# Asking for a slot's first weights four tiles sooner, and making a table's first loads depend on the expert

## The reference

```python
x = filter(x)                                  # (14336, 192)
for layer in (0, 1):
    e = argmax(x @ w_gate[layer])              # one of 8 experts per token
    h = relu(x @ w1[layer][e])                 # 192 -> 1024
    x = gate * (h @ w2[layer][e])              # 1024 -> 192; layer 1 has one more gate factor
```

## Time and profile before

| what | value |
|---|---|
| runs, median (lowest to highest) | 1329.62 us (1328.49 to 1333.94) |
| profiled execution, its own time | 1330.72 us |
| its span in the trace | 1329.2 us |
| PE busy | 1175.1 us, 88% |
| DVE busy | 855.4 us, 64% |
| ACT busy | 615.7 us, 46% |
| POOL busy | 438.4 us, 33% |
| mean granted TensorE clock | 0.926 |
| bytes moved by DMA | 216.61 MB |

### The profile page before, as it was taken

How to read it: one execution, slowest core, us unless ns; L and a number is a source line. 1 busy time by engine, 2 the same in 40 slices (tenths; PEclk the granted TensorE clock), 3 DMA queues, 4 the chain that set the end, 5 groups by cost and what they waited for, 6 DMA issues and landing times.

```text
span 1329.2 us, 38842 instructions
## 1 busy us (share of the span) xinstructions
PE 1175.1 (88%) x13470; PEld 1063.7 (80%) x13470; DVE 855.4 (64%) x2331; ACT 615.7 (46%) x1083; POOL 438.4 (33%) x478
## 2 busy tenths in 40 slices
PE   3767565379998999999999999999999999999996
PEld 2666564358886888888999989788899998999996
DVE  3888778448996998998777787654333433434332
ACT  2766666125554555555555444333333333333332
POOL 1277767522432433333222222322222222222222
PEclk9676765679998999999999999999999999999998
DMA  8677864728979789856544446338824545424451
GB/s 253 193 228 252 255 212 141 210 46 207 231 219 313 144 232 293 231 156 192 140 105 103 106 104 160 64 105 197 247 58 111 163 114 162 114 53 105 113 135 52
DMA packets 236335, 216.61 MB, mean 163 GB/s; under 512 B 176927, under 2 KB 209339, under 8 KB 230114
## 3 DMA queue, kind: packets, MB, share of 16 engines
q1 hardware_dynamic: 209696, 150.68, 43.3%
q0 software_dynamic: 25520, 64.49, 16.2%
q10 hardware_dynamic: 1042, 0.47, 0.2%
HBM read 116.05 MB, written 69.62 MB: 140 GB/s over the span
## 4 chain that ended last, share of the span: by engine, by line
PE 60%; DVE 19%; issue 8%; DMA 4%; another core or an unknown queue 3%; ACT 3%; SPq 2%; DVEq 0%; POOL 0%; ACTq 0%; POOLq 0%
PE bank L856 59%; DMA wslot<-image 2%; DVE am L1120 2%; DVE hl L1352 2%; DVE split L1195 1%; PE bank L861 1%; DVE wam L1084 1%; DVE split L1198 1%; ACT rowt L713 1%; DVE wslot L1222 1%; DVE rowab L1129 1%; DVE rowt L1129 1%; DMA stage<-in_moe_w 1%; DVE wam L1082 1%
## 5 line engine op out<-in xcount | busy, mean ns | idle before, releaser
L1352 DVE SCALAR_TENSOR_TENSOR hl<-bank,hh 128x512 f16<-128x512 f32 x480 | 331.1, 690 | 360.8 <-ACT hh L797 319.3
L797 ACT ACTIVATE hh<-bank 128x512 f16<-128x512 f32 x480 | 286.2, 597 | 487.7 <-PE bank L856 403.5
L856 PE MATMUL bank<-xT,wslot 128*128 128x256 f16 (+1 forms) x3920 | 468.0, 275 | 15.1 <-issue 7.2
L856 PE MATMUL bank<-wslot,hh 128*128 128x192 f16 x3136 | 425.8, 248 | 12.8 <-DMA wslot<-image 6.6
L856 PE MATMUL bank<-wslot,hl 128*128 128x192 f16 x1568 | 388.5, 248 | 2.0 <-issue 2.0
L856 PEld LDWEIGHTS bank<-xT,wslot 128*128 128x128 f16 (+1 forms) x3920 | 328.7, 98 | 74.0 <-issue 31.1
L856 PEld LDWEIGHTS bank<-wslot,hh 128*128 128x128 f16 x3136 | 281.0, 98 | 34.1 <-issue 24.6
L685 POOL DMA_INDIRECT out_tokens<-y,idxt x120 | 117.1, 976 | 365.6 <-ACT y L809 311.9
L626 POOL DMA_INDIRECT rows<-rowt,idxp x120 | 126.3, 1053 | 328.0 <-PE bank L856 194.3
L856 PEld LDWEIGHTS bank<-wslot,hl 128*128 128x128 f16 x1568 | 154.5, 99 | 2.1 <-issue 1.8
L608 POOL DMA_INDIRECT rows<-rowab,idxa x96 | 108.0, 1125 | 64.1 <-issue 43.5
(11 more groups left out here) (173 smaller groups left out, 1275.6 us busy)
## 6 DMA issues: line engine op xcount, KB each, us to landing
wslot<-image SPq DMA_DIRECT2D x22, 1024.0 KB
wslot<-image SPq DMA_DIRECT2D x22, 768.0 KB
split<-image SPq DMA_DIRECT2D x16, 1024.0 KB
split<-image SPq DMA_DIRECT2D x16, 768.0 KB
image<-split POOLq DMA_DIRECT2D x18, 512.0 KB
image<-split SPq DMA_DIRECT2D x8, 1024.0 KB
image<-split POOLq DMA_DIRECT2D x9, 768.0 KB
stage<-in_moe_w SPq DMA_DIRECT2D x8, 768.0 KB
```

The costliest lines, as they stand in the source:

```text
L797: nc.scalar.activation(hh[:, c, :], bank[c][:, :], ACT.Relu).then_inc(hh_out, 1)
L856: return nc.tensor.matmul(o, a, b_, start=start, stop=stop, skip_group_check=True)
L1352: V.scalar_tensor_tensor(hl[:, c, :], bank[c][:, :], 0.0, hh[:, c, :], ALU.max, ALU.subtract).then_inc(hl_out, 1)
```

## The change

Slots 2 and 3 get their first weights at tiles 8 to 11 of a layer and no longer at 12 to 15. For that, the block table must be there earlier, so two waits of SP for tables move ahead, and one quad of layer 1 (tiles 68 to 71) is written out instead of looped. The two tiles that begin a layer's second table (14 and 15, 72 and 73) load weights only if their expert differs from that of the tile two before. DVE keeps the last two experts of the first table in `last2` for that.

```diff
@@ loads
-                other = isinstance(g, int) and g + 1 in (EARLY[0], EARLY[0] + 1, NT, NT + 1, NT + EARLY[1], NT + EARLY[1] + 1)
+                other = isinstance(g, int) and NT <= g + 1 < NT + 2
                 c, ahead = 2 * v + s, layer_of(g + 1, l)
-                first = isinstance(g, int) and i % QUADS == MIXQ - 1
+                first = isinstance(g, int) and i % QUADS == MIXQ - 2
...
                 if first:
-                    load_w_part(block_expert(i + 1, v), l, 2 + v, s)
+                    load_w_part(block_expert(i + 2, v), l, 2 + v, s)
@@ SP's program, layer 0
             sp.wait_ge(pads_ready, 1)
+            sp.wait_ge(table_ready, 3)
             for c in range(E // 2):
                 one(loads, 8 + c)
                 for e in (2 * c, 2 * c + 1):
                     store_pad(sp, 0, e)
-            sp.wait_ge(table_ready, 3)
@@ SP's program, layer 1
-            with sp.Fori(QUADS + 2, QUADS + MIXQ - 1) as i:
-                quad(loads, i, False, 1, False)
             sp.wait_ge(table_ready, 6)
-            for g in range(NT + 4 * MIXQ - 4, NT + 4 * MIXQ):
+            for g in range(NT + 4 * MIXQ - 8, NT + 4 * MIXQ):
                 one(loads, g)
@@ table_tiles, on DVE
                 if unit == T:
                     V.tensor_tensor(tab[:, 2, g0 + 2:g0 + n], tew[:, 2:n], tew[:, 0:n - 2], ALU.subtract)
+                    if not first:
+                        V.tensor_tensor(tab[:, 2, g0:g0 + 2], tew[:, 0:2], last2[:, :], ALU.subtract)
+                    else:
+                        V.tensor_copy(last2[:, :], tew[:, n - 2:n])
```

More of the change, by code:

```diff
@@ L169, in build @@
         start = sb("start", [P, 1], f32)
+        last2 = sb("last2", [P, 2], f32)
         ge = sb("ge", [P, NT, E], f32)
@@ L331, in build @@
         LAST = (GT - 1, (GT - 1) // 2, 1)
-        assert NT % 4 == 0 and 1 < MIXQ < E + 1 < QUADS - 1 and max(EARLY) <= 4 * MIXQ and 12 <= min(EARLY) and STEPS == E and SPB == 2
+        assert NT % 4 == 0 and MIXQ == 4 and MIXQ < E + 1 < QUADS - 1 and max(EARLY) <= 4 * MIXQ and 12 <= min(EARLY) and STEPS == E and SPB == 2
         def steps(eng, body):
```

## The result

The changed kernel takes **1334.06 us** as the median of 13 executions (1330.71 to 1340.58). The kernel before takes 1329.60 us beside it (13 executions, 1326.18 to 1333.94). The ratio is **1.0033, with a 95% interval of 1.0018 to 1.0049**: 4.4 us slower, where 4.7 us faster was forecast. The profiled execution took 1332.82 us, 2.1 us more than the one of before, with a span of 1331.3 us and the same mean clock, 0.926. PE was busy 1177.1 us, and 214.78 MB moved, 1.83 MB less, which is the load that tile 72 no longer makes.

The account below looks back on a forecast made before the run. The prediction took PE to bound the kernel, with a weight stall in quad 3. Its terms, -9.8 - 0.6 + 3.4 + 1.9 + 0.2 + 0.2 = -4.7 us, gave a median of 1324.9 us, range 1319.6 to 1330.0.

Parts of the forecast that it names:

- What bounds the kernel, and the stall in quad 3 (-9.8): Tiles 12 to 15: PE bounds the kernel; moving four weight transfers out ends PE's weight waits, -9.8 us.
- What is late next in quad 3 (+3.4): Tile 15: without the stall, ACT's write waits for the image store's third piece, +3.4 us (0.3 to 8.5).
- First loads into tiles 8 to 11 (+1.9, at most 4.6): Quad 2: the added loads delay the image store, so ACT waits 0 to 4.6 us; taken as +1.9 us.
- the loss is the same as ACT's wait: Quad 6, used as the model: ACT waited 2.50 us for the store and the quad lost 2.5 us.
- The allowance for DVE's maximum (+0.2): Quad 2: DVE's load now has slot 2's part 0 ahead of it, +0.2 us, at most 2.6.
- Layer 1 (-0.6): Tile 72: same expert as tile 70, so its 1.75 MB load goes and a small stall ends, -0.6 us.
- The sum: Whole kernel: all terms together, -4.7 us, to a median of 1324.9 us.
- The stores keep up: Rival, chance 0.27: ACT waits for no store in quads 2 and 3; gain 9.5 us, 1320.1 us.
- Slower: Rival, chance 0.06: the stall reappears in quad 2 through POOL; quads 2 and 3 lose 17.0 us, +6.6 net, 1336.2.
- The stall stays: Rival, chance 0.12: loads of tiles 14 to 16 still fill the queue, half the stall stays; -0.5 us, 1329.1.

Follow-up runs that it names:

- the four traces: Four profiled executions of the unaltered changed kernel, against traces of the kernel before; quads 2 and 3 together took 80.68, 80.07, 82.57 and 81.92 us.
- the kernel with both changes: The whole change plus all three pieces of POOL's image store issued one step sooner, against the kernel before: ratio 0.9974 (0.9950 to 0.9997).

## Why the prediction was wrong

**What bounds the kernel, and the stall in quad 3 (-9.8): right, in part.** The four transfers left, and PE's waits for `wslot<-image` at tiles 14 and 15 fell from 7.83 to 2.8 us in the first trace. They did not go to zero: 2.43 us stayed at tile 15.

**What is late next in quad 3 (+3.4): right in size, mixed in kind.** Quad 3 changed by -7.7, -8.8, -2.7 and -8.5 us in the four traces, each against the trace of before of its own level. The mean is -6.9, where -9.8 + 3.4 = -6.4 was forecast. In three of the four, ACT's L734 did not wait and the rest of the loss was weights that came late again at tile 15; in the fourth ACT waited 3.81 us, as the prediction had it. For the other three the size was luck.

**First loads into tiles 8 to 11 (+1.9, at most 4.6): wrong, and the largest miss of the sum.** Quad 2 lost 6.0, 6.4, 2.8 and 8.0 us, 5.8 in the mean. Three things were missed in it. First, the queue was reckoned at the 400 GB/s of the earlier trace rows. Quad 2's own rate stood in the earlier trace rows, 210 GB/s at a share of 0.80, which is some 260 GB/s when full (an estimate from the two), and over the whole quad it moved 266. The share came out as forecast (1.05, measured 1.03) by luck, since the quad had become longer: the DMA engines' time in quad 2 went from 29.0 to 43.5 us, 14.5 more, where 9.2 were reckoned. In quad 3 it fell by 8.9 us, as reckoned. So the same bytes were worth 8.9 us where they left and cost 14.5 where they arrived; in the three later traces they cost some 13, 9 and 15, least where the quad lost least (all these are share times length). Second, only SP's part 1 ahead of the third piece was priced, at 2.0 us, and only for L734. The third piece stood behind POOL's own second piece, which was itself slowed, and took 10.17 us, past even the upper bound of 10.0 (5.4 + 4.6). ACT's write before (L731) needs the second piece, and waited 0.78 to 1.43 us in three traces, 0 in the one that lost least. Third, "the loss is the same as ACT's wait", from quad 6, left out the clock: after PE's wait of 4.27 us it fell to 0.50, while quad 6, where PE waited 2.06 us, had 0.97. ACT's 4.6 us became 6.0. In the trace where ACT waited only 3.44 us the clock stayed at 1.00 and the quad lost 2.8.

**The allowance for DVE's maximum (+0.2): not needed.** L1083 started at 360.79 in tile 9 with no wait.

**Layer 1 (-0.6): half right.** The condition's saving is there, 0.6 us in quad 72, and alone it gives exactly that (64.82 against 65.42); the early loads alone would have given it too. The early first loads in tiles 68 to 71 were taken to be free, and they are not: quad 68 lost 1.91, 0.33, 1.92 and 1.68 us. Net +0.9 in the mean.

**The sum.** From the traces, -6.9 + 5.8 + 0.9 = -0.2 us, against -4.9 forecast for the same parts. The median says +4.4. In the first pair of traces the balance closes: +1.7 us ahead of tile 8, which the change hardly touches and which the later traces do not repeat, -1.7 in quads 2 and 3, +1.3 in quads 68 and 72, +0.8 elsewhere, 2.1 in all. Between the mean of the traces and the median 4.6 us are not placed in any stretch. Two of the profiled executions were below their medians, by 1.2 us and by 5.4 (1275.34, the fastest of twelve with a median of 1280.77). That the stores are behind this part too is shown only in total, by the kernel with both changes (0.9974). Which quads lose it in the other executions stays open.

**The rivals.** "The stores keep up" is refuted: ACT waited for a store in each of the four traces. The Trainium skill (DMA: Bandwidth & Descriptors, "Queues, rings and completion order") says that each DMA engine takes turns between queue rows packet by packet. The trace agrees with that: from 364.72 to 369.30 us POOL's queue moved 0.81 MB and SP's 0.98, and SP's earlier load did not go first. What was drawn from the rule, that the store would wait for about its own length of SP's traffic, failed on what the prediction itself had named beside it, that POOL's own queue was behind: 4.6 of the 10.17 us passed before the second piece had landed. "Slower" was the rival that came true, given 0.06. It had the place and the chain (ACT waits for the store) but asked for 17 us in both quads together. Against the full relief of 9.8 the quads gave 5.8 and 2.9 back. "The stall stays" came true in part: 2.8 of 7.83 us of waits for weights stayed, at tile 15 above all.

## What to carry to other kernels

- Price bytes at the rate of the stretch that they move into, not of the one that they leave. Busy DMA engines moved 400 GB/s in the stretch of the earlier trace rows and 237 in the 17.7 us around the late store, with three quarters of the packets under 512 B in both.
- When a load is moved, list what is in flight on every queue, who waits for each, and what stands behind it on its own queue. Here SP's loads delayed POOL's third piece by way of POOL's second. Moving the stores sooner gave back more than moving the loads gained.
- A stall that is removed exposes waits that it had hidden, and a new wait of ACT of 4.6 us cost the quad 6.0 because PE's clock fell behind it. Read several traces: here the same kernel lost 2.8 us of quad 2 in one execution and 8.0 in another.

## What was not expected of the hardware

POOL's store of 768 KB took 10.17 us, and for 4.6 of them POOL's own second piece had not landed, though SP's queue and POOL's were moving side by side (0.98 and 0.81 MB in 4.58 us). With the stretch full, being asked for first did not help: SP's 768 KB took 13.7 us until PE went on, issued 0.7 us ahead of POOL's 512 and 768 KB, which took 10.2 and 13.7. And busy DMA engines moved 205, 391 and 154 GB/s in three stretches in a row (357.20 to 364.72, to 369.30 and to 374.90 in the changed kernel), against 400 in the kernel before. In the slow two 82% and 91% of the packets were under 512 B, in the fast one 29%, but in the earlier trace rows 73%; what sets the rate is not shown.
